# Gated linear attention in front of two MLPs: chunk decay moved onto q, weight splits moved to VectorE, y summed in two ways

## The chip, the cores and the metric

The kernel runs on one core of a Trainium2 chip. A core has TensorE (matrix products into PSUM; the profile calls its products PE and its weight loads PEld), VectorE (DVE), ScalarE (ACT), GpSimd (POOL) and SyncE (SP, here only a queue for transfers). The metric is device time in microseconds for one execution, and smaller is better.

## The reference

Shapes are batch 4, 8 heads, 768 positions and head width 48. The attention's output goes as 3072 tokens of 384 numbers through two MLPs in turn, with hidden widths 1536 and 2048. All inputs are 32-bit floats.

```python
f = 1.0 / (1.0 + np.exp(-f_logit))
for t in range(S):
    state = f[:, :, t, :, None] * state + np.einsum('bhd,bhe->bhde', k[:, :, t], v[:, :, t])
    y[:, :, t] = np.einsum('bhd,bhde->bhe', q[:, :, t], state)
# y as (3072 tokens, 384) is x of the first MLP, whose result is x of the second
gate = 1.0 / (1.0 + np.exp(-(x @ w_gate)));  x = gate * (x @ w_val) @ w_out
h = x @ w_in;  out = h * (1.0 / (1.0 + np.exp(-1.702 * h))) @ w_out
```

## The kernel before

**Attention in chunks.** The work is cut into 48 units. A unit is two heads and 256 positions, in four chunks of 64 positions. `Unit(n).third` says which third of the 768 positions it is, and a first third has no state ahead of it. For each unit the gates are multiplied up within a chunk (`prod`), q is multiplied by that product (`q_dec`) and k by its reciprocal (`k_dec`). Then y of a chunk is the masked scores `q_dec` times `k_dec` applied to v, plus `q_dec` times the state that stood ahead of the chunk. `p_end` is the product at a chunk's last position.

**Visits.** TensorE does the attention in 53 visits of small products. A visit turns one unit (transposes `k_dec` and makes its scores), makes the products of k and v of the unit before it (`kept`, at KV_COL of the banks), and makes y of the unit before that (`made`): the scores' part at Y_COL, the states' part at STATE_COL. Eight visits (BEFORE_MLP) stand ahead of the first MLP block; there both parts of y are summed in PSUM at Y_COL, which needs a wait of TensorE for its own earlier products (`tiles_done`). The other 45 stand inside MLP blocks, as the table VISIT_AT says: in blocks 1, 2, 4, 6, 8 of group 0 and in blocks 0, 1, 3, 4, 5, 7, 8, 9 of groups 1 to 5. PREPARE_AT does the same for the making of `prod`, its reciprocal, `q_dec` and `k_dec`, and FORGET_AT for the gates.

**MLP blocks.** The first MLP runs over seven groups of tokens: groups 0 and 1 have 256 tokens, the others 512, and each has 12 blocks of 128 hidden units. Each product is made as three, of parts that are rounded to fp32r (`w_hi`, `x_hi`) and of remainders (`w_lo`, `x_lo`), so every weight has to be split once. For block q, TensorE makes the gate (bank 0 of `up_ps`) and the value (bank 1), then the visit, if the block has one, and then the output product of block q-1. ScalarE takes the sigmoid of the gate (line 695), VectorE multiplies it by the value (line 891), ScalarE rounds that (`act_hi`, line 701) and VectorE takes the remainder (`act_lo`, line 900). Bank 0 of the next block waits for the sigmoid, bank 1 for the product, and the output product waits for the remainder. The second MLP follows in six groups of 512 tokens and 16 blocks each.

**Order.** Every engine runs an order that is written out by hand. In a block with a visit, VectorE goes on with `after_visit`: the mask of the scores (line 802), then `new_states`, which first multiplies all four chunks' k and v products by `p_end` from PSUM (line 812, it releases `kv_done`) and then adds the decayed state chunk by chunk (line 820). ScalarE in that block copies `k_rows` (line 616), takes y (`take_y`: four copies of the states' part, line 630, and one of the scores' part, line 633), makes the gates of a later unit (`forget`, lines 597 and 598) and, in group 0, rounds a piece of the first MLP's weights (line 578). GpSimd makes `q_dec` and `k_dec` (lines 509 and 514), adds the two parts of y (line 534) and splits the odd pieces 3, 5, 7, 9 and 11 of the weights (line 528); VectorE splits pieces 1, 2, 4, 6, 8 and 10 (line 842). SyncE's queue loads q, k, v and the gates' inputs and moves y into `x_raw` (line 402), from which the next group's x is split.

## Time and profile before

| | us |
|---|---|
| median of 3 runs | 967.32 |
| the runs | 965.22, 967.32, 1544.05 |
| the profiled execution, its own time | 964.99 |
| its span in the trace | 963.3 |
| TensorE busy | 934.1 (97%) |
| VectorE busy | 493.7 (51%) |
| ScalarE busy | 349.5 (36%) |
| GpSimd busy | 152.4 (16%) |

All times of rows are microseconds from the start of the span. In the rows of a timeline come start, duration, engine, line, operation, tile written and tiles read, and in brackets how long the engine had been idle and what ended it. Small matrix products overlap on TensorE, so its busy time is no measure of a full array. The columns of a window are its length, then the busy time and count of PE, PEld, DVE, ACT and POOL, then the granted share of TensorE's clock, the share of the DMA engines and their GB/s. The windows below are cut at the starts of VectorE's product of gate and value (line 891): 36.48, 44.24 and 90.27 are those of blocks 1, 2 and 10 of group 0; 95.82 and 142.66 those of blocks 0 and 10 of group 1; 181.94 and 189.57 those of blocks 4 and 5, and 197.19 and 203.31 those of blocks 6 and 7 of group 2. 149.43 is the first product of group 2.

### The profile page before, as it was taken

The numbers are of one execution on the slowest core, as the hardware profiler recorded it, in microseconds if no ns is written. First come the engines' busy times: TensorE is split into PE (matmuls) and PEld (weight loads), VectorE is DVE, ScalarE is ACT, GpSimd is POOL, SyncE is SP. The second block draws the span as 40 slices with busy tenths as digits, with TensorE's granted clock in tenths as the row PEclk, the third lists the DMA queues.
The fourth block names the chain that finished last, engine by engine and source line by source line (L and its number), as shares of the span: only waits on it lengthen the run. The fifth ranks groups of instructions, "written<-read, shape, count | busy, mean of one in ns | idle before, by whom it ended". The sixth has DMA issues, their size and how long they took to land.

```text
span 963.3 us, 18025 instructions
## 1 busy us (share of the span) xinstructions
PE 934.1 (97%) x7219; PEld 781.0 (81%) x7219; DVE 493.7 (51%) x872; ACT 349.5 (36%) x797; POOL 152.4 (16%) x174
## 2 busy tenths in 40 slices
PE   7888998999999999999999999999999999999997
PEld 5777897888888888888888888888888888888885
DVE  8976867655655765565333234343343443443433
ACT  3454453343434433333324333333332233233332
POOL 4443332221221221112004430000000000000000
PEclk9989999999999999999999999999999999999999
DMA  6642232211221211121032330020010100100000
GB/s 162 181 141 67 74 81 70 59 44 43 75 62 51 67 52 52 44 71 30 21 107 68 97 115 1 1 66 0 1 66 1 54 13 1 65 1 1 33 1 35
DMA packets 44007, 52.35 MB, mean 54 GB/s; under 512 B 8464, under 2 KB 33808, under 8 KB 43920
## 3 DMA queue, kind: packets, MB, share of 16 engines
q1 hardware_dynamic: 41184, 43.30, 15.5%
q10 hardware_dynamic: 2736, 7.85, 2.8%
q8 instruction: 59, 0.97, 0.4%
q14 instruction: 28, 0.23, 0.1%
HBM read 36.96 MB, written 9.44 MB: 48 GB/s over the span
## 4 chain that ended last, share of the span: by engine, by line
PE 85%; DVE 6%; issue 3%; ACT 2%; SPq 2%; DMA 1%; POOL 0%; ACTq 0%; DVEq 0%; POOLq 0%
PE up_ps L1052 16%; PE up_ps L1054 16%; PE up_ps L1053 16%; PE out_ps L1052 12%; PE out_ps L1053 11%; PE out_ps L1054 11%; PE att_ps L1003 1%; DVE prod L782 1%; SPq L402 1%; DVE act_lo L900 1%; DVE w_lo L842 1%; PE att_ps L1025 1%; PE att_ps L1045 1%; DVE inv_prod L789 1%; PE att_ps L1015 1%
## 5 line engine op out<-in xcount | busy, mean ns | idle before, releaser
L1052 PE MATMUL up_ps<-x_hi,w_hi 128*128 128x512 f32 (+1 forms) x792 | 295.1, 373 | 13.3 <-ACT act_f L695 12.1
L1054 PE MATMUL up_ps<-x_hi,w_lo 128*128 128x512 f32 (+1 forms) x792 | 294.5, 372 | 0.0
L1053 PE MATMUL up_ps<-x_lo,w_hi 128*128 128x512 f32 (+1 forms) x792 | 294.4, 372 | 0.0
L1052 PE MATMUL out_ps<-act_hi,w_hi 128*128 128x512 f32 (+1 forms) x540 | 208.6, 386 | 1.1 <-DVE act_lo L900 1.1
L1053 PE MATMUL out_ps<-act_lo,w_hi 128*128 128x512 f32 (+1 forms) x540 | 203.5, 377 | 0.0
L1054 PE MATMUL out_ps<-act_hi,w_lo 128*128 128x512 f32 (+1 forms) x540 | 203.1, 376 | 0.0
L701 ACT CAST act_hi<-act_f 128x512 fp32r<-128x512 f32 (+1 forms) x180 | 106.6, 592 | 249.6 <-DVE act_f L891 177.1
L900 DVE TENSOR_TENSOR act_lo<-act_f,act_hi 128x512 fp32r<-128x512 f32 (+1 forms) x180 | 126.1, 700 | 116.0 <-ACT act_hi L701 116.0
L1052 PEld LDWEIGHTS up_ps<-x_hi,w_hi 128*128 128x128 f32 x792 | 150.6, 190 | 40.1 <-issue 10.9
L1054 PEld LDWEIGHTS up_ps<-x_hi,w_lo 128*128 128x128 f32 x792 | 150.8, 190 | 25.4
L1053 PEld LDWEIGHTS up_ps<-x_lo,w_hi 128*128 128x128 f32 x792 | 150.8, 190 | 25.1
L894 DVE TENSOR_TENSOR act_f<-act_f,up_ps 128x512 f32<-128x512 f32 x96 | 66.1, 688 | 173.3 <-ACT act_f L697 173.3
L891 DVE TENSOR_TENSOR act_f<-act_f,up_ps 128x512 f32<-128x512 f32 (+1 forms) x84 | 51.2, 609 | 162.4 <-PE up_ps L1054 149.7
L697 ACT ACTIVATE act_f<-up_ps 128x512 f32<-128x512 f32 x96 | 57.4, 598 | 192.9 <-PE up_ps L1054 192.9
L1052 PEld LDWEIGHTS out_ps<-act_hi,w_hi 128*128 128x128 f32 x540 | 102.2, 189 | 22.8 <-DVE act_lo L900 1.8
L1054 PEld LDWEIGHTS out_ps<-act_hi,w_lo 128*128 128x128 f32 x540 | 102.3, 189 | 18.7
L1053 PEld LDWEIGHTS out_ps<-act_lo,w_hi 128*128 128x128 f32 x540 | 102.4, 190 | 17.0
L789 DVE RECIPROCAL inv_prod<-prod 128x256 f32<-128x256 f32 x48 | 84.1, 1753 | 1.6
L695 ACT ACTIVATE act_f<-up_ps 128x512 f32<-128x512 f32 (+1 forms) x84 | 45.0, 535 | 84.2 <-PE up_ps L1054 84.2
L630 ACT COPY y_t<-att_ps 48x128 f32<-48x128 f32 x176 | 45.8, 260 | 55.2 <-DVE state L812 53.6
L534 POOL TENSOR_TENSOR y_t<-y_t,y_scores 128x256 f32<-128x256 f32 x44 | 32.3, 734 | 210.4 <-ACT y_scores L633 210.4
L820 DVE SCALAR_TENSOR_TENSOR state<-state,p_end 128x48 f32<-128x48 f32 x176 | 47.7, 271 | 6.2
(77 smaller groups left out, 581.0 us busy)
## 6 DMA issues: line engine op xcount, KB each, us to landing
stage<-w SPq DMA_DIRECT2D x16, 384.0 KB, 3.3
stage<-w ACTq DMA_DIRECT2D x9, 576.0 KB, 4.3
q_raw<-q_t SPq DMA_DIRECT2D x96, 48.0 KB, 1.9
k_raw<-k_t SPq DMA_DIRECT2D x96, 48.0 KB, 1.9
v_raw<-v_n SPq DMA_DIRECT2D x48, 96.0 KB, 2.2
x_raw<-x_dram SPq DMA_DIRECT2D x6, 768.0 KB, 4.7
out_t<-final SPq DMA_DIRECT2D x18, 256.0 KB, 2.3
f_raw<-f_t SPq DMA_DIRECT2D x82, 48.0 KB, 1.9
```

The source lines that it names most:

```text
L630: act.copy(y[rows[i], :, r, :], banks(v)[rows[r], i, STATE_COL:STATE_COL + BLOCKS * C].rearrange("p (c t) -> p c t", c=BLOCKS))
L695: act.activation(act_f[:, b.t, 0:b.n], up_ps[:, 0, 0:b.n], ACT.Sigmoid).then_inc(sig_done, 1)
L697: act.activation(act_f[:, b.t, 0:b.n], up_ps[:, b.j % 2, 0:b.n], ACT.Sigmoid, scale=1.702).then_inc(sig_done, 1)
L701: act.copy(act_hi[:, b.t, 0:b.n], act_f[:, b.t, 0:b.n]).then_inc(act_hi_done, 1)
L789: dve.reciprocal(inv_prod[:, u.s, :], prod[:, u.s, :]).then_inc(inv_done, 1)
L820: dve.scalar_tensor_tensor(out=after[:, c, :], in0=state_before(u, c), scalar=p_end[:, n, c:c + 1], in1=after[:, c, :], op0=ALU.mult, op1= ...
L891: dve.tensor_tensor(act_f[:, b.t, 0:b.n], act_f[:, b.t, 0:b.n], up_ps[:, 1, 0:b.n], ALU.mult).then_inc(mul_done, 1)
L894: dve.tensor_tensor(act_f[:, b.t, 0:b.n], act_f[:, b.t, 0:b.n], up_ps[:, b.j % 2, 0:b.n], ALU.mult).then_inc(mul_done, 1)
L900: dve.tensor_tensor(act_lo[:, b.t, 0:b.n], act_f[:, b.t, 0:b.n], act_hi[:, b.t, 0:b.n].bitcast(F32), ALU.subtract).then_inc(act_split, 1)
L1052: pe.matmul(dst, w_hi[:, at:at + P], m_hi, start=first, stop=False)
L1053: pe.matmul(dst, w_hi[:, at:at + P], m_lo, start=False, stop=False)
L1054: return pe.matmul(dst, w_lo[:, at:at + P], m_hi, start=False, stop=last)
```

## The change

Four things change.

1. A state is now kept without the decay of its own chunk. `new_states` no longer multiplies the k and v products by `p_end`; each chunk's step reads them from PSUM and adds the state before it times the decay of the chunk before (`end_before`). The missing factor is put on q: ScalarE makes `q_in` from `q_dec`, chunk by chunk (`prepare_q`), and TensorE multiplies states by `q_in`. ScalarE also copies `p_end` now (`take_end`), which VectorE did.
2. VectorE splits all pieces of the first MLP's weights but the first; GpSimd's `split_w1_piece` goes.
3. For the visits of groups 0 and 1 (ahead of `APART`) TensorE sums both parts of y at Y_COL, as it did before the first block, behind its wait for `tiles_done`. ScalarE takes y in one copy, which no longer waits for VectorE; VectorE waits for that copy before it masks the scores (`copied_first`).
4. From group 2 on ScalarE makes the four copies of the states' part, once the states are done, and VectorE adds the scores' part from PSUM (`add_y`), where GpSimd did.

Some pieces of the order ahead of the first block are moved too: ScalarE rounds weight pieces 1 and 2 later, behind the copies of y and behind the first x; GpSimd makes unit 4's `k_dec` behind its last third of piece 0; SyncE loads the gates' input of unit 8 ahead of q and k of unit 7.

```diff
+
+    APART = VISIT_AT[2, 0]
...
+        def copied_first(v):
+
+            return BEFORE_MLP <= v < APART
 
         def wait_y(eng, n):
 
-            if out_visit[n] < BEFORE_MLP:
-                eng.wait_ge(y_taken, n + 1)
+            if out_visit[n] < APART:
+                eng.wait_ge(y_copied, n + 1)
             else:
-                eng.wait_ge(y_added, n - UG + 1)
+                eng.wait_ge(y_added, len([m for m in range(n + 1) if out_visit[m] >= APART]))
...
+        def end_before(u, c):
+
+            return p_end[:, u.n, c - 1:c] if c else p_end[:, u.n - UG, CH - 1:CH]
...
-                def split_w1_piece(t):
-
-                    piece = slice(t * PIECE1, (t + 1) * PIECE1)
-                    pool.wait_ge(w1_hi_done, t + 1)
-                    pool.tensor_tensor(w_lo[:, piece], w1_staged(t), w_hi[:, piece].bitcast(F32),
-                                       ALU.subtract).then_inc(w1_pool_split, 1)
-
-                def add_y(n):
-
-                    pool.wait_ge(y_taken, n + 1)
-                    pool.tensor_tensor(y_t[:, n % YS, :], y_t[:, n % YS, :], y_scores[:, n % 2, :], ALU.add).then_inc(y_added, 1)
...
-                pool.wait_ge(state_done, states_before(2))
+                pool.wait_ge(state_done, CH * 2)
                 split_w1(0)
                 split_w1(1)
-                decay(4)
+                decay_q(4)
+                pool.wait_ge(state_done, CH * 4)
                 split_w1(2)
+                decay_k(4)
...
                 for g in range(NG1 - 1):
                     for j in range(J1):
-                        if g == 0 and j + 2 < J1 and by_pool(j + 2):
-                            split_w1_piece(j + 2)
-                        if (g, j) in VISIT_AT and VISITS[VISIT_AT[g, j]][2] is not None:
-                            add_y(VISITS[VISIT_AT[g, j]][2])
                         if (g, j) in PREPARE_AT:
+                def take_end(n):
+
+                    act.wait_ge(scan_done, n + 1)
+                    act.copy(p_end[:, n, :],
+                             prod[:, n % 2, :].rearrange("p (c t) -> p c t", c=CH)[:, :, C - 1]).then_inc(p_end_done, 1)
+
+                def prepare_q(n):
+
+                    u = Unit(n)
+                    act.wait_ge(q_dec_done, n + 1)
+                    if n >= 2:
+                        act.wait_ge(visit_done, out_visit[n - 2] + 1)
+                    act.wait_ge(p_end_done, n + 1)
+                    for c in range(0 if u.third else 1, CH):
+                        at = slice(c * C, (c + 1) * C)
+                        last = act.mul(q_in[:, n % 2, at], q_dec[:, n % 4, at], end_before(u, c))
+                    last.then_inc(q_in_done, 1)
+
                 def take_y(n):
                     v = out_visit[n]
                     act.wait_ge(visit_done, v + 1)
-                    wait_products_read(act, v)
+                    if not copied_first(v):
+                        wait_products_read(act, v)
                     wait(act, y_moved[n % YS], 16 * moves(n % YS, n))
-                    scores_part = banks(v)[:, :, Y_COL:STATE_COL].rearrange("p r (c t) -> p c r t", c=BLOCKS)
                     y = y_t[:, n % YS, :].rearrange("p (c r t) -> p c r t", c=BLOCKS, r=SIDES)
-                    if v < BEFORE_MLP:
-                        act.copy(y, scores_part).then_inc(y_taken, 1)
+                    if v < APART:
+                        act.copy(y, banks(v)[:, :, Y_COL:STATE_COL].rearrange("p r (c t) -> p c r t", c=BLOCKS)).then_inc(y_copied, 1)
                         return
                     for i in range(PAIR):
                         for r in range(SIDES):
-                            act.copy(y[rows[i], :, r, :], banks(v)[rows[r], i, STATE_COL:STATE_COL + BLOCKS * C].rearrange(
+                            last = act.copy(y[rows[i], :, r, :], banks(v)[rows[r], i, STATE_COL:STATE_COL + BLOCKS * C].rearrange(
                                 "p (c t) -> p c t", c=BLOCKS))
-                    wait(act, y_added, n - 1 - UG)
-                    act.copy(y_scores[:, n % 2, :].rearrange("p (c r t) -> p c r t", c=BLOCKS, r=SIDES),
-                             scores_part).then_inc(y_taken, 1)
+                    last.then_inc(y_copied, 1)
...
+                    turned = made = None
                     if b.first_mlp and (b.g, b.j) in VISIT_AT:
                         turned, _, made = VISITS[VISIT_AT[b.g, b.j]]
-                        if turned is not None:
-                            take_k(turned)
-                        if made is not None:
-                            take_y(made)
+                    if turned is not None:
+                        take_k(turned)
+                        take_end(turned)
+                    if made is not None:
+                        take_y(made)
+                    if turned is not None:
+                        prepare_q(turned)
...
                     after = states_of(u)
-                    dve.tensor_tensor(after.rearrange("p (c r) e -> p r c e", r=SIDES),
-                                      banks(v)[:, :, KV_COL:Y_COL].rearrange("p r (c e) -> p r c e", c=BLOCKS),
-                                      p_end[:, n, :].rearrange("p (c r) -> p r c", r=SIDES).unsqueeze(3).to_broadcast(
-                                          [P, SIDES, BLOCKS, D]), ALU.mult).then_inc(kv_done, 1)
-                    dve.wait_ge(kv_done, n + 1)
-                    for m, c in enumerate(range(0 if u.third else 1, CH)):
-                        if m:
-                            dve.wait_ge(state_done, states_before(n) + m)
-                        dve.scalar_tensor_tensor(out=after[:, c, :], in0=state_before(u, c), scalar=p_end[:, n, c:c + 1],
-                                                 in1=after[:, c, :], op0=ALU.mult, op1=ALU.add).then_inc(state_done, 1)
+                    for c in range(CH):
+                        products = banks(v)[:, c % SIDES, KV_COL + c // SIDES * D:KV_COL + (c // SIDES + 1) * D]
+                        if c:
+                            dve.wait_ge(state_done, CH * n + c)
+                        if c == 0 and not u.third:
+                            dve.tensor_copy(after[:, c, :], products).then_inc(state_done, 1)
+                        else:
+                            dve.scalar_tensor_tensor(out=after[:, c, :], in0=state_before(u, c), scalar=end_before(u, c),
+                                                     in1=products, op0=ALU.mult, op1=ALU.add).then_inc(state_done, 1)
+
+                def add_y(n, v):
+
+
+                    dve.wait_ge(y_copied, n + 1)
+                    y = y_t[:, n % YS, :].rearrange("p (c r t) -> p r c t", c=BLOCKS, r=SIDES)
+                    dve.tensor_tensor(y, y, banks(v)[:, :, Y_COL:STATE_COL].rearrange("p r (c t) -> p r c t", c=BLOCKS),
+                                      ALU.add).then_inc(y_added, 1)
 
                 def after_visit(v):
                     turned, kept, made = VISITS[v]
                     dve.wait_ge(visit_done, v + 1)
+                    if made is not None and copied_first(v):
+                        wait_y(dve, made)
                     if turned is not None:
                         mask(turned, v)
                     if kept is not None:
                         new_states(kept, v)
+                    if made is not None and v >= APART:
+                        add_y(made, v)
...
                         if before[1] is not None:
-                            pe.wait_ge(kv_done, before[1] + 1)
+                            pe.wait_ge(state_done, CH * (before[1] + 1))
                         if before[2] is not None:
-                            pe.wait_ge(y_taken, before[2] + 1)
+                            wait_y(pe, before[2])
...
-                    if made is not None and v < BEFORE_MLP:
+                    if made is not None and v < APART:
 
                         last.then_inc(tiles_done, 1)
                         pe.wait_ge(tiles_done, made + 1)
-                        pe.wait_ge(state_done, states_before(made + 1))
+                        pe.wait_ge(state_done, CH * (made + 1))
+                        pe.wait_ge(q_in_done, made + 1)
                         for c in range(0 if m.third else 1, CH):
                             at = slice(Y_COL + c // SIDES * C, Y_COL + (c // SIDES + 1) * C)
                             for i in range(PAIR):
                                 last = pe.matmul(ps[rows[i], c % SIDES, at], state_before(m, c)[rows[i], :],
-                                                 q_dec[rows[i], made % 4, c * C:(c + 1) * C], start=False, stop=False,
+                                                 q_in[rows[i], made % 2, c * C:(c + 1) * C], start=False, stop=False,
                                                  skip_group_check=True)
                     elif made is not None:
 
-                        pe.wait_ge(state_done, states_before(made + 1))
+                        pe.wait_ge(state_done, CH * (made + 1))
+                        pe.wait_ge(q_in_done, made + 1)
                         for c in range(CH):
                             at = slice(STATE_COL + c // SIDES * C, STATE_COL + (c // SIDES + 1) * C)
+                            q = q_in[:, made % 2, c * C:(c + 1) * C] if m.third or c else q_dec[:, made % 4, 0:C]
                             for i in range(PAIR):
-                                last = pe.matmul(ps[rows[c % SIDES], i, at], state_before(m, c)[rows[i], :],
-                                                 q_dec[rows[i], made % 4, c * C:(c + 1) * C], start=False, stop=False,
+                                last = pe.matmul(ps[rows[c % SIDES], i, at], state_before(m, c)[rows[i], :], q[rows[i], :],
+                                                 start=False, stop=False,
```

The blocks 2 and 3 of group 0 on VectorE, from one product of gate and value to the last operation ahead of block 4's, in the kernel before:

```order
L891 TENSOR_TENSOR act_f<-act_f,up_ps 128x256
L842 TENSOR_TENSOR w_lo<-stage,w_hi 128x1152
L900 TENSOR_TENSOR act_lo<-act_f,act_hi 128x256
L802 TENSOR_TENSOR scores<-att_ps,causal 128x256
L812 TENSOR_TENSOR state<-att_ps,p_end 128x2x2x48
L820 SCALAR_TENSOR_TENSOR state<-state,p_end 128x48 x4
L891 TENSOR_TENSOR act_f<-act_f,up_ps 128x256
L900 TENSOR_TENSOR act_lo<-act_f,act_hi 128x256
L782 SCALAR_TENSOR_TENSOR prod<-gate,floor 128x256
L789 RECIPROCAL inv_prod<-prod 128x256
L790 COPY p_end<-prod 128x4
```

and in the changed kernel:

```order
L923 TENSOR_TENSOR act_f<-act_f,up_ps 128x256
L874 TENSOR_TENSOR w_lo<-stage,w_hi 128x1152
L932 TENSOR_TENSOR act_lo<-act_f,act_hi 128x256
L822 TENSOR_TENSOR scores<-att_ps,causal 128x256
L840 SCALAR_TENSOR_TENSOR state<-state,p_end,att_ps 128x48 x4
L923 TENSOR_TENSOR act_f<-act_f,up_ps 128x256
L874 TENSOR_TENSOR w_lo<-stage,w_hi 128x1152
L932 TENSOR_TENSOR act_lo<-act_f,act_hi 128x256
L804 SCALAR_TENSOR_TENSOR prod<-gate,floor 128x256
L811 RECIPROCAL inv_prod<-prod 128x256
```

The product of the states with `p_end` and the copy of `p_end` are gone, and block 3 has a split of a weight piece.

The same block 2 on ScalarE, from the rounding of `act_f` to the sigmoid of block 3, before:

```order
L701 CAST act_hi<-act_f 128x256
L616 COPY k_rows<-turn_ps 128x256
L630 COPY y_t<-att_ps 48x2x64 x4
L633 COPY y_scores<-att_ps 128x256
L597 ACTIVATE gate<-f_raw 128x4x63
L598 ACTIVATE floor<-f_raw 128x4
L578 CAST w_hi<-stage 128x1152
L572 DMA final<-w 128x1152
L695 ACTIVATE act_f<-up_ps 128x256
```

and changed:

```order
L718 CAST act_hi<-act_f 128x256
L607 COPY k_rows<-turn_ps 128x256
L612 COPY p_end<-prod 128x4
L635 COPY y_t<-att_ps 128x256
L624 ACTIVATE q_in<-q_dec,p_end 128x64 x4
L588 ACTIVATE gate<-f_raw 128x4x63
L589 ACTIVATE floor<-f_raw 128x4
L569 CAST w_hi<-stage 128x1152
L563 DMA final<-w 128x1152
L712 ACTIVATE act_f<-up_ps 128x256
```

Five copies of y have become one, and a copy of `p_end` and four products that make `q_in` stand behind it.

TensorE in the visit of block 2, with what each instruction waits for, before:

```order
L982 MATMUL turn_ps<-ident,k_dec 128x128 [waits k_rows_done,k_dec_done]
L982 MATMUL turn_ps<-ident,k_dec 128x128
L1003 MATMUL att_ps<-scores,v_raw 48x64 [waits scores_masked,kv_done]
L1003 MATMUL att_ps<-scores,v_raw 48x64 x7
L1015 MATMUL att_ps<-v_raw,k_rows 64x48 [waits v_loaded1,k_rows_done]
L1015 MATMUL att_ps<-v_raw,k_rows 64x48 x7
L1025 MATMUL att_ps<-q_dec,k_dec 64x64 [waits q_dec_done]
L1025 MATMUL att_ps<-q_dec,k_dec 64x64 x7
L1045 MATMUL att_ps<-q_dec,state 48x64 [waits state_done]
L1045 MATMUL att_ps<-q_dec,state 48x64 x7
```

and changed:

```order
L1014 MATMUL turn_ps<-ident,k_dec 128x128 [waits k_rows_done,k_dec_done]
L1014 MATMUL turn_ps<-ident,k_dec 128x128
L1035 MATMUL att_ps<-scores,v_raw 48x64 [waits scores_masked,state_done]
L1035 MATMUL att_ps<-scores,v_raw 48x64 x7
L1047 MATMUL att_ps<-v_raw,k_rows 64x48 [waits v_loaded1,k_rows_done]
L1047 MATMUL att_ps<-v_raw,k_rows 64x48 x7
L1057 MATMUL att_ps<-q_dec,k_dec 64x64 [waits q_dec_done]
L1057 MATMUL att_ps<-q_dec,k_dec 64x64 x7
L1069 MATMUL att_ps<-q_in,state 48x64 [waits q_in_done,state_done,tiles_done]
L1069 MATMUL att_ps<-q_in,state 48x64 x7
```

The last eight products now wait for TensorE's own earlier ones and for `q_in`, and the first ones for the finished states and not for `kv_done`.

## Rows read from the trace of the kernel before

**Rows 1.** The page, part 1: busy time, share of the span, instructions.

```profile
PE 934.1 (97%) x7219; PEld 781.0 (81%) x7219; DVE 493.7 (51%) x872; ACT 349.5 (36%) x797; POOL 152.4 (16%) x174
```

**Rows 2.** Windows: us; PE, PEld, DVE, ACT, POOL busy (count); PEclk; DMA; GB/s.

```profile
36.48:44.24 7.76, 5.18 (x87) 4.50 (x87) 7.11 (x12) 2.51 (x6) 4.08 (x4) 0.86 0.50 141
44.24:90.27 46.03, 36.87 (x418) 35.07 (x418) 34.74 (x58) 21.42 (x55) 19.46 (x16) 0.87 0.38 108
95.82:142.66 46.84, 45.04 (x801) 42.64 (x800) 35.87 (x85) 23.40 (x82) 14.45 (x20) 1.00 0.28 75
149.43:963.30 813.87, 807.78 (x5418) 665.85 (x5418) 375.73 (x649) 282.72 (x605) 96.06 (x106) 1.00 0.14 43
181.94:189.57 7.63, 7.63 (x95) 6.25 (x93) 5.43 (x12) 3.31 (x10) 2.17 (x3) 1.00 0.26 69
197.19:203.31 6.12, 6.12 (x29) 4.93 (x27) 3.76 (x5) 1.22 (x2) 1.47 (x2) 1.00 0.26 65
```

**Rows 3.** Timeline of VectorE, blocks 4 and 5: start, us, engine, line, operation.

```profile
55.75 0.42 DVE L891 TENSOR_TENSOR act_f<-act_f,up_ps 128x256 f32<-128x256 f32 x1
56.08 1.83 DVE L842 TENSOR_TENSOR w_lo<-stage,w_hi 128x1152 fp32r<-128x1152 f32 x1
57.83 0.41 DVE L900 TENSOR_TENSOR act_lo<-act_f,act_hi 128x256 fp32r<-128x256 f32 x1
58.17 0.41 DVE L802 TENSOR_TENSOR scores<-att_ps,causal 128x256 f32<-128x256 f32 x1
58.50 0.34 DVE L812 TENSOR_TENSOR state<-att_ps,p_end 128x192 f32<-128x192 f32 x1
58.87 1.18 DVE L820 SCALAR_TENSOR_TENSOR state<-state,p_end 128x48 f32<-128x48 f32 x4
...
63.12 1.80 DVE L900 TENSOR_TENSOR act_lo<-act_f,act_hi 128x256 fp32r<-128x256 f32 x1 [0.47 <-ACT act_hi L701]
64.85 0.68 DVE L782 TENSOR_TENSOR_SCAN prod<-gate,floor 128x256 f32<-128x256 f32 x1
65.56 1.75 DVE L789 RECIPROCAL inv_prod<-prod 128x256 f32<-128x256 f32 x1
```

**Rows 4.** Timeline of ScalarE in block 4, up to the sigmoid of block 5.

```profile
56.51 0.37 ACT L616 COPY k_rows<-turn_ps 128x256 f32<-128x256 f32 x1
59.00 1.08 ACT L630 COPY y_t<-att_ps 48x128 f32<-48x128 f32 x4 [2.12 <-DVE state L812]
...
60.68 0.20 ACT L598 ACTIVATE floor<-f_raw 128x4 f32<-128x4 f32 x1
60.77 1.14 ACT L578 CAST w_hi<-final 128x1152 fp32r<-128x1152 f32 x1
61.82 0.38 ACT L695 ACTIVATE act_f<-up_ps 128x256 f32<-128x256 f32 x1
```

**Rows 5.** Timeline of GpSimd in blocks 4 and 5.

```profile
55.95 0.74 POOL L514 TENSOR_TENSOR k_dec<-k_raw,inv_prod 128x256 f32<-128x256 f32 x1 [1.06 <-issue]
...
61.99 2.65 POOL L528 TENSOR_TENSOR w_lo<-final,w_hi 128x1152 fp32r<-128x1152 f32 x1 [0.72 <-ACT w_hi L578]
```

**Rows 6.** Timeline of weight loads at the third visit, ahead of the first block.

```profile
14.78 0.39 PEld L1036 LDWEIGHTS att_ps<-q_dec,state 48*48 48x48 f32 x12 [0.23 <-PE att_ps L1025]
```

**Rows 7.** Timeline of ScalarE while the first x comes in.

```profile
26.89 1.15 ACT L578 CAST w_hi<-stage 128x1152 fp32r<-128x1152 f32 x1 [2.25 <-DMA stage<-w]
```

**Rows 8.** Timeline of SyncE's queue at the end of group 1.

```profile
145.93 1.16 SPq L402 DMA_DIRECT2D x_raw<-y_t  x2
```

**Rows 9.** Timeline of ScalarE there: the last third of group 2's x.

```profile
148.47 0.62 ACT L647 CAST x_hi<-x_raw 128x512 fp32r<-128x512 f32 x1 [3.80 <-DMA x_raw<-y_t]
```

**Rows 10.** Timeline of TensorE there, groups 1 to 2.

```profile
146.47 0.28 PE L1053 MATMUL out_ps<-act_lo,w_hi 128*128 128x256 f32 x1
146.59 0.28 PE L1054 MATMUL out_ps<-act_hi,w_lo 128*128 128x256 f32 x1
149.43 0.50 PE L1052 MATMUL up_ps<-x_hi,w_hi 128*128 128x512 f32 x1 [2.56 <-ACT act_f L695]
```

52 lines of the change are left out of this document (29 added, 23 removed).

## The prediction

> **What bounds the kernel now.** I read the page's busy shares first, then windows cut at VectorE's product of gate and value, then the timelines of the engines inside one window. TensorE is busy 97% of the span [rows 1], so an edit elsewhere pays only where TensorE waits. The windows show where that is. From 149.43 us to the end TensorE is busy 807.8 of 813.9 us [rows 2]; there a block with a visit takes 7.63 us and one without 6.12, both fully busy, so a visit costs TensorE 1.51 us [rows 2]. A block of 256 tokens is 27 products that start 0.12 us apart [rows 10], 3.24 us. From 44.24 to 90.27 TensorE has eight such blocks and at most four visits, 8 x 3.24 + 4 x 1.51 = 32.0 us of work in a window of 46.03 us [rows 2]. That window, the one ahead of it (7.76 us) and the wait at 149.43 are where this change can move the end.
>
> Two blocks of group 0 take 46.03 / 4 = 11.5 us. The loop goes through VectorE and ScalarE. VectorE multiplies at 55.75, splits weights, takes the remainder at 57.83, masks, multiplies the k and v products by the decay, and starts the states at 58.87 [rows 3]. ScalarE can copy y only after that multiplication, at 59.00; then come 1.77 us of copies and gates and a weight cast of 1.05 us, so the next sigmoid starts at 61.82 [rows 4]. The product that follows it is 6.5 us behind the one at 55.75. In the next block VectorE's remainder takes 1.80 us, where the one before it left room for the mask after 0.34 [rows 3]: GpSimd was splitting a weight piece from 61.99 to 64.64 [rows 5], and the scan started at 64.85, when it was done.
>
> **Group 0, blocks 2 to 9.** I lay out the two blocks anew from the product M of the block with the visit. VectorE: weight split at M + 0.33, remainder at + 2.08, mask at + 2.42 [rows 3]. The multiplication of the k and v products is gone, so the four state steps start at + 2.75 and take 1.1 us, to + 3.85. They now read PSUM; the nearest row is the multiplication that did, 0.34 us for 192 elements, against 1.18 / 4 = 0.3 for a step of 48 [rows 3], so I add nothing, and 0.05 each at most. ScalarE: `k_rows` at + 0.76 [rows 4], then the copy of `p_end` (0.1), one copy of y (0.27), at + 1.4 the four products for `q_in`. No row shows these. From below they cost 0.1 each, the step from the small gate at 60.68 to the cast at 60.77; from above I take 0.5, twice a copy of y, which is 1.08 / 4 = 0.27 [rows 4]. I take 0.27, as small operations in a row with separate operands are nearest to it. Then gates 0.42 (1.77 less four copies and the fifth of 0.27), cast 1.05, sigmoid 0.4 [rows 4]: the next product comes at + 4.4, and ScalarE, not VectorE's + 3.85, paces it.
>
> The Trainium skill, "ScalarE: Activation LUTs", section "What ACT_TABLE_LOAD costs", says that each operand given as a pointer of one element a partition adds about 93 ns to an ACTIVATE, and that ACTIVATEs in a row overlap by as much; that makes an estimate of 0.24 us for each of the four, and 0.1 us less per two blocks than my sum. No row here shows it.
>
> The second block has no visit: product 0.33, split 1.2, remainder 0.34, scan 0.70, reciprocal 1.7 [rows 3] = 4.25 us. The split is priced from the row at 56.08: it lasts 1.83 us, but GpSimd's `k_dec` ran until 55.95 + 0.74 = 56.69 [rows 5], and 57.91 - 56.69 = 1.2 is left. GpSimd does nothing at that point of the second block now, so 1.2 stands, and 1.83 is the bound from above. Sum 8.6 us against 11.5, and for four such pairs a gain of **11.6 us**. TensorE's floor, 2 x 3.24 + 1.51 + 0.23 (below) = 8.2, lies just under it, so no more than 13 can be had here.
>
> The Trainium skill, "SBUF — State Buffer", section "Who interferes with whom", speaks against moving such work: a VectorE instruction with two inputs in SBUF and a GpSimd instruction that reads SBUF lock each other out for a whole instruction. By that rule the new splits still collide with `q_dec` and `k_dec`, and if each of the five met one the four pairs would gain 9 and not 11.6. The trace agrees that there is such a collision (1.83 against 1.2, and 1.80 against a remainder's 0.41 [rows 3]), but those products follow the scan and the reciprocal, which in the second block come after the split.
>
> **Group 0, the ends.** Between the products of blocks 1 and 2 lie 7.76 us [rows 2], with the same stall by GpSimd. Laid out anew: 2.42 to the mask, 0.33, 1.1 of states, 0.7 of scan, 1.7 of reciprocal = 6.25, a gain of **1.5**. From block 10's product to the first one of group 1 there are 5.55 us [rows 2]; TensorE needs 0.42 until the product is done, four times 1.08 us, and 0.3 for the last to land, 5.05. The clock was below full for part of the window just before (mean 0.87), and with TensorE kept busy I expect it back: **0.5**.
>
> **Ahead of the first block.** ScalarE waited 2.25 us for a weight piece and only then copied `k_rows` and rounded x [rows 7]. The piece now comes behind x. But y is copied later, since for it the states must be finished, and the products for `q_in` lengthen ScalarE's way to the first sigmoid. I take **0.4** of gain, between a loss of 1 and a gain of 1.5 (the 1.15 us of the cast and a little of the wait).
>
> **Group 1.** Ten blocks and eight visits take 46.84 us [rows 2]. TensorE now waits for its own products in each visit. At a visit that already did, its weight load sat idle 0.23 us for that [rows 6]. Its floor becomes 10 x 3.24 + 8 x (1.51 + 0.23) = 46.3. VectorE's loop there loses the multiplication, which put 0.37 us ahead of the states [rows 3], and gains a wait for the copy of y ahead of the mask: with no split in the block the mask could start 1.2 us behind the product, and ScalarE, by the layout above, is through with y at about 1.55, 0.35 later. So blocks with a visit and a preparation stay as long as they are, and those with a visit alone get shorter, since ScalarE comes to the next sigmoid earlier. The floor binds: **0.5**, with 0 to -5 if the two waits add up (rival 2). At its end TensorE is through its products at 146.7 and starts group 2 at 149.43, 2.56 us idle [rows 10]: ScalarE's third rounding of x waited until 148.47 for a transfer [rows 9] that SyncE issued at 145.93, without a pause behind the one before it [rows 8], so the queue itself was late. Each y is ready about 2.6 us earlier now: 1.1 for four copies of the five, 0.7 for GpSimd's sum (priced as `k_dec` [rows 5]), 0.8 for ScalarE's wait for VectorE. A queue that fills up behind y ends about as much earlier. VectorE's split of x then follows its reciprocal, which keeps 0.7 us: **1.9**.
>
> **Groups 2 to 5** have 32 visits. GpSimd's sum goes, VectorE's comes. VectorE's blocks: scores at 2.42 less 0.34 behind the remainder plus 0.65 for 512 columns, states done at about 3.4 from the product, wait 1.1 for ScalarE's four copies, sum 0.34, scan 0.7, reciprocal 1.7: 7.3 us in a block of 7.63. It fits, TensorE stays full, and nothing moves. If that cover is gone, see rival 3. The rest has no edit.
>
> **Sum.** 0.4 + 1.5 + 11.6 + 0.5 + 0.5 + 1.9 = 16.4 us from the profiled execution's 964.99 (span 963.3): 948.6. The two ordinary runs lie 0.2 and 2.3 above that execution, so for a median I take **949.5**. About 2%, 19.3 us, is what a measurement of this kernel can tell from no change.
>
> **Rivals.** (1) ScalarE and GpSimd pace group 0. If the four products take 0.5 each, the next product comes at + 5.3 and the pair at 9.5 us: the gain shrinks by 3.6, and with every split locked out by GpSimd, 1.83 in both blocks, by 2.5 more, to about 10.3: 955.5. For it: its chain holds 3.9 us of the 4.4 already. Against: a gate of 4 columns costs it 0.1. (2) In group 1 VectorE's wait for the copy (0.35) and TensorE's own wait (0.23) come in series, eight times, 4.6 us, and 0.5 is not gained: 11.3 in all, 954.5. For it: both engines are within 0.5 us of each other there. (3) The other side: groups 2 to 5. VectorE's 7.3 us rest on a wait for ScalarE. If copies, `q_in` and sum cost 0.8 us more a visit than counted, a block takes 8.1, 0.5 over TensorE's, and 32 visits give back 16: 965.5. At 1.4 more it is 984, slower than before. It decides from 7.63 us on, and only if the blocks without a visit don't catch up; TensorE runs 4.9 us (1.51 + 2 x 2.04 - 0.7) behind the product before it feels it, which speaks against it. (4) Both loops reach TensorE's floor and the start gains its 1.5: 13 + 1.5 + 1.5 + 0.5 + 0.5 + 2.6 = 19.6: 945.5. (5) The change doesn't do what it says in group 0: the sigmoid stays late because the early copy of y waits for a visit that TensorE ends late, and only the stalls by GpSimd go (1.8 - 0.4 less the split's 1.2): next to nothing there, 963.
>
> **How the numbers follow.** Forecast 0.58 (946.5 to 952.5), rival 1 0.12, rival 2 0.09, rival 3 0.04 (0.03 over 2%), rival 4 0.15, rival 5 0.02. The range 945 to 957.5 takes in the forecast, 1, 2 and 4 with the bounds of the unknown costs, and leaves out 3, 5 and tails of the others. Faster by over 2% needs 948.0 or less against the median, which rival 4 gives and the forecast's lower end against one reading of the two runs: 0.25. Slower by over 2%: 0.03. Within: 0.72.
>
> **What would show it.** The pair of blocks in group 0 at 8.6 us (8.2 if TensorE binds, 9.5 if rival 1); no remainder of 1.8 us on VectorE; `q_in` products near 0.3 us; group 1's window at 46 to 47 and not 50; the idle ahead of group 2 below 0.8; blocks of group 2 still 7.63 and 6.12; the clock at 2.4 GHz through most of group 0. The forecast is wrong if TensorE waits in groups 2 to 5, or if the first product of group 0 starts more than 1 us from 31.3.

## The result: 953.13 us, 13 us less than before

The changed kernel takes 953.13 us (median of five, 952.64 to 954.03), the kernel before 966.21 beside it; the ratio of the two is 0.9868, with a 95% interval of 0.9852 to 0.9883. That is a gain of 1.3%, inside the 2% that was set for "no change", and 3.6 us above the forecast of 949.5. One of the five executions of the kernel before stood at 1544 us; the median counts it, the ratio leaves it out. The profiled execution took 953.08 us with a span of 951.0, against 964.99 and 963.3.

The page of the changed kernel, part 1 [beside rows 1]:

```profile
PE 934.9 (98%) x7203; PEld 781.2 (82%) x7203; DVE 487.0 (51%) x829; ACT 375.3 (39%) x941; POOL 105.8 (11%) x125
```

VectorE has 7 us less to do, ScalarE 26 more, GpSimd 47 less, and TensorE the same. So the 12.3 us between the spans are waits of TensorE that are gone. Where they were is seen in windows of the changed kernel, cut at VectorE's product of gate and value as in [rows 2] (columns: us; busy us and count of PE, PEld, DVE, ACT, POOL; granted clock; DMA share; GB/s):

```profile
0.00:34.60 34.60, 27.18 (x354) 20.66 (x354) 25.02 (x45) 17.03 (x53) 13.13 (x25) 0.95 0.64 178
...
39.05:45.27 6.22, 4.66 (x89) 4.24 (x88) 6.08 (x12) 3.57 (x11) 1.47 (x2) 0.96 0.57 161
45.27:79.52 34.25, 33.99 (x425) 32.84 (x424) 32.36 (x53) 21.27 (x59) 5.85 (x8) 0.96 0.51 146
...
84.84:132.68 47.84, 47.14 (x785) 44.21 (x784) 33.62 (x75) 22.89 (x86) 8.80 (x12) 1.00 0.31 82
132.68:137.08 4.40, 4.21 (x36) 4.03 (x35) 3.89 (x6) 2.25 (x5) 1.29 (x2) 1.00 0.25 66
137.08:951.00 813.92, 808.04 (x5418) 665.86 (x5418) 379.08 (x630) 303.74 (x715) 73.22 (x75) 1.00 0.15 43
```

Set against the windows of before, this is the whole account:

```
stretch                                   before   after   gain   forecast
start to the first product                 31.72   34.60   -2.9      0.4
product of block 0 to 1                     4.76    4.45    0.3      0
product of block 1 to 2                     7.76    6.22    1.5      1.5
blocks 2 to 10 of group 0 (four pairs)     46.03   34.25   11.8     11.6
block 10 to group 1                         5.55    5.32    0.2      0.5
group 1, ten blocks, eight visits          46.84   47.84   -1.0      0.5
to TensorE's start of group 2               6.77    4.40    2.4      1.9
groups 2 to 5, and the rest               813.87  813.92    0        0
sum                                                        12.3     16.4
```

A pair of blocks now takes 34.25 / 4 = 8.56 us. That is a mean: in the first block of the four pairs TensorE's clock was granted at 0.67 and the block took 4.45 us,

```profile
45.27:49.72 4.45, 4.45 (x29) 4.45 (x28) 3.80 (x9) 3.73 (x12) 0.73 (x1) 0.67 0.40 103
```

and the other three pairs took 8.49 us (4.16 behind the block with the visit, 4.33 behind the other). In the run with one slab in the gap, below, the clock was full in all four pairs, and they took 33.96 us, 8.49 each. VectorE's timeline in blocks 6 and 7 [beside rows 3]:

```profile
62.54 0.36 DVE L923 TENSOR_TENSOR act_f<-act_f,up_ps 128x256 f32<-128x256 f32 x1
62.82 1.88 DVE L874 TENSOR_TENSOR w_lo<-stage,w_hi 128x1152 fp32r<-128x1152 f32 x1
64.62 0.41 DVE L932 TENSOR_TENSOR act_lo<-act_f,act_hi 128x256 fp32r<-128x256 f32 x1
64.95 0.41 DVE L822 TENSOR_TENSOR scores<-att_ps,causal 128x256 f32<-128x256 f32 x1
65.29 1.15 DVE L840 SCALAR_TENSOR_TENSOR state<-state,p_end,att_ps 128x48 f32<-128x48 f32 x4
66.70 0.42 DVE L923 TENSOR_TENSOR act_f<-act_f,up_ps 128x256 f32<-128x256 f32 x1 [0.26 <-ACT act_f L712]
67.04 1.35 DVE L874 TENSOR_TENSOR w_lo<-stage,w_hi 128x1152 fp32r<-128x1152 f32 x1
...
```

The multiplication of the k and v products is gone, and so is the remainder of 1.80 us. VectorE idles 0.26 us in the pair, where ScalarE's sigmoid comes last. The second split meets no GpSimd instruction and takes 1.35 us; the first meets `k_dec` and takes 1.88. ScalarE's timeline in the same pair [beside rows 4]:

```profile
63.24 0.37 ACT L607 COPY k_rows<-turn_ps 128x256 f32<-128x256 f32 x1
...
63.61 0.38 ACT L635 COPY y_t<-att_ps 128x256 f32<-128x256 f32 x1
63.87 0.36 ACT L624 ACTIVATE q_in<-q_dec,p_end 128x64 f32<-128x64 f32 x1
...
64.12 0.82 ACT L624 ACTIVATE q_in<-q_dec,p_end 128x64 f32<-128x64 f32 x3
64.84 0.41 ACT L588 ACTIVATE gate<-f_raw 128x252 f32<-128x252 f32 x1
...
65.24 1.15 ACT L569 CAST w_hi<-stage 128x1152 fp32r<-128x1152 f32 x1
66.28 0.39 ACT L712 ACTIVATE act_f<-up_ps 128x256 f32<-128x256 f32 x1
```

y is copied 1.07 us behind the product, where it was 3.25 [rows 3, 4], in one copy and not five. TensorE's list of waits says the same. Of the kernel before (engine, line, what is waited for: us in total, times, longest):

```profile
PE up_ps L1052 <- ACT act_f L695: 12.1, 7, 2.7
```

and of the changed one:

```profile
PE out_ps L1035 <- DVE state L840: 2.4, 1, 2.4
...
PE up_ps L1087 <- ACT act_f L712: 0.6, 1, 0.6
```

The 12.1 us take in the 2.56 us ahead of group 2 [rows 10]. The wait of 2.4 us stands ahead of the first block. It is longer than before and not new: in the same visits of the kernel before TensorE waited 0.80 us for the copy of y (at 20.89) and 0.23 and 0.41 us for states (at 21.57 and 22.75), 1.4 us in all. ScalarE's timeline there, where y of pairs 0 to 3 is copied at 18.32, 22.34, 24.67 and 25.96 (17.14, 20.27, 22.15 and 24.28 in the kernel before):

```profile
18.32 0.37 ACT L635 COPY y_t<-att_ps 128x256 f32<-128x256 f32 x1 [0.98 <-DVE state L840]
...
18.95 0.83 ACT L624 ACTIVATE q_in<-q_dec,p_end 128x64 f32<-128x64 f32 x3
19.68 0.40 ACT L588 ACTIVATE gate<-f_raw 128x252 f32<-128x252 f32 x1
...
22.34 0.37 ACT L635 COPY y_t<-out_ps 128x256 f32<-128x256 f32 x1 [2.16 <-DVE state L838]
```

VectorE's scan of that gate stands ahead of its mask of the fourth visit (its second row is the mask of 20.82):

```profile
20.21 0.69 DVE L804 TENSOR_TENSOR_SCAN prod<-gate,floor 128x256 f32<-128x256 f32 x1 [2.00 <-ACT floor L589]
20.82 0.40 DVE L822 TENSOR_TENSOR scores<-out_ps,causal 128x256 f32<-128x256 f32 x1
```

SyncE moves y into x, one transfer behind the other, from the second copy of y on: from 22.74 and not from 20.85. And TensorE ran at half its clock for a while: the 16 small products that fill the time ahead of pair 4's transposition took 2.05 us in the kernel before (granted clock 1.00),

```profile
23.22 2.05 PE L967 MATMUL up_ps<-ident 128*128 128x128 f32 x16
```

and in the changed kernel, with 0.50 from 25.0 to 27.0 (1.2 GHz),

```profile
25.16 3.25 PE L999 MATMUL up_ps<-ident 128*128 128x128 f32 x16
```

### The profile page after: what moved, and what is told of

The parts are those of the page before. It is cut to its first block, busy times and chain, and to the rows that moved or that the text cites. A ratio compares the mean times of both kernels' runs of the same rounds, so it can differ in the third digit from the quotient of the medians.

```text
span 951.0 us, 18139 instructions
## 1 busy us (share of the span) xinstructions
PE 934.9 (98%) x7203; PEld 781.2 (82%) x7203; DVE 487.0 (51%) x829; ACT 375.3 (39%) x941; POOL 105.8 (11%) x125
## 4 chain that ended last, share of the span: by engine, by line
PE 95%; DVE 2%; issue 1%; ACT 1%; DMA 1%; SPq 0%; ACTq 0%; POOL 0%; DVEq 0%; POOLq 0%
PE up_ps L1087 17%; PE up_ps L1088 17%; PE up_ps L1089 17%; PE out_ps L1087 13%; PE out_ps L1088 12%; PE out_ps L1089 12%; PE att_ps L1035 2%; PE att_ps L1057 1%; PE att_ps L1047 1%; PE turn_ps L1014 1%; PE up_ps L1003 1%; PE att_ps L1069 1%; PE att_ps L1080 1%; DMA x_raw<-y_t 1%; DVE inv_prod L811 1%
## 5 line engine op out<-in xcount | busy, mean ns | idle before, releaser
L932 DVE TENSOR_TENSOR act_lo<-act_f,act_hi 128x512 fp32r<-128x512 f32 (+1 forms) x180 | 118.1, 656 | 113.8 <-ACT act_hi L718 113.8
L506 POOL TENSOR_TENSOR q_dec<-q_raw,prod 128x256 f32<-128x256 f32 x48 | 35.3, 735 | 299.6 <-DVE prod L804 229.9
L639 ACT COPY y_t<-att_ps 48x128 f32<-48x128 f32 x128 | 33.3, 260 | 60.3 <-DVE state L840 59.2
L624 ACT ACTIVATE q_in<-q_dec,p_end 128x64 f32<-128x64 f32 x176 | 47.4, 339 | 0.9
```

The source lines that it names most:

```text
L506: pool.tensor_tensor(q_dec[:, n % 4, :], q_raw[:, u.s, :], prod[:, u.s, :], ALU.mult).then_inc(q_dec_done, 1)
L624: last = act.mul(q_in[:, n % 2, at], q_dec[:, n % 4, at], end_before(u, c))
L932: dve.tensor_tensor(act_lo[:, b.t, 0:b.n], act_f[:, b.t, 0:b.n], act_hi[:, b.t, 0:b.n].bitcast(F32), ALU.subtract).then_inc(act_split, 1)
```

## The experiments

The theory after the result had four parts. (1) The early copy of y carries the gain of group 0, since it takes VectorE's work out of ScalarE's way. (2) The splits' move carries a small part of it. (3) The 2.9 us lost at the start come of the order of ScalarE's queue. (4) Group 1 loses 1.0 us to TensorE's wait for its own products. The rivals stand with each run. The runs bear out (1), and (2) with a size of 0.7 us a pair. They bear out (3) only in part and (4) only in part, as is said where they stand.

**Splits back on GpSimd.** The diff against the changed kernel; `split_w1_piece`, `by_pool` and the semaphore are as in the kernel before:

```
+                        if g == 0 and j + 2 < J1 and by_pool(j + 2):
+                            split_w1_piece(j + 2)
...
-                    if b.q < J1 and b.j + 2 < J1:
+                    if b.q < J1 and b.j + 2 < J1 and not by_pool(b.j + 2):
```

> The changed kernel with one part undone: every second split of a weight piece goes back to GpSimd. Theory A (a GpSimd split stops VectorE's two-input instructions while it runs, so moving it to VectorE is part of the gain): GpSimd's 2.65 us from about 0.3 us ahead of the product hold up the remainder and the scan of the second block of each pair; the pair goes from 8.56 to about 9.3, and blocks 1 to 2 from 6.22 to 7: 957 against 953.1. Theory B (the split's owner doesn't matter, only the multiplication of the k and v products and the four copies did): VectorE has 1.35 us less in a pair whose two blocks take 4.16 and 4.33, TensorE's 8.3 binds: 952, 1 us less. In both the start and group 1 stay as they are, within 0.5.

Measured: 954.08 us (953.34 to 954.4). Four pairs took 36.78 us, 9.20 each. The timelines of GpSimd, and then of VectorE, in the second block of a pair:

```profile
66.52 2.68 POOL L540 TENSOR_TENSOR w_lo<-stage,w_hi 128x1152 fp32r<-128x1152 f32 x1 [2.97 <-ACT w_hi L585]
```

```profile
67.65 1.84 DVE L948 TENSOR_TENSOR act_lo<-act_f,act_hi 128x256 fp32r<-128x256 f32 x1 [0.47 <-ACT act_hi L734]
```

The remainder of 1.84 us is back; GpSimd's split ends at 69.20 and the remainder at 69.49. Theory A in mechanism and in the length of the pair. The pairs are 2.5 us longer than in the changed kernel's profile, and 2.8 us, 0.7 a pair, longer than four pairs of 8.49. The time rose by 1.0 us and not by 4: the pairs cost 2.5 and not 3, blocks 1 to 2 nothing (6.03 us) where I expected 0.8, and this execution's first product came 0.8 us earlier, for a reason that the table below shows.

**Gates first.** ScalarE's order ahead of the first block:

```
+                forget(4)
                 w1_first_part(0)
                 take_y(0)
                 take_end(3)
                 take_k(3)
-                load_w1(1)
                 prepare_q(2)
-                forget(4)
-                take_y(1)
-                prepare_q(3)
+                load_w1(1)
                 first_load_f(6)
                 load_w1(2)
                 forget(5)
+                prepare_q(3)
+                take_y(1)
                 take_y(2)
```

> The changed kernel with ScalarE's order ahead of the first block changed: the gate of pair 4 ahead of the rounding of the first weight piece and of the copy of y of pair 0, and the gate of pair 5, the load of f of pair 6, the load of weight piece 2 and q_in of pair 3 ahead of the copy of y of pair 1. Theory A (the first block starts 2.9 us later than before because ScalarE's q_in products and the later copies of y stand ahead of a gate whose scan in turn stands ahead of VectorE's mask): the mask of the fourth visit comes at about 20.0 instead of 20.8, TensorE's wait of 2.38 us at 22.97 falls below 1.7, the copies of y of pairs 2 and 3 at about 23.3 and 24.5 instead of 24.67 and 25.96, and the first product at 33.1 to 33.4 instead of 34.60: 951.4 to 952. Theory B (it is late because y needs the finished states and the warm-up ended 1.2 us later in that execution; the gates only fill time): the first product stays at 34.3 to 34.7 and the time at 953.

Measured: 952.01 us (950.4 to 952.3), first product at 33.72. The mask came at 19.33, but y of pair 1 was copied at 21.83, behind the gate and `q_in` that I had moved ahead of it, and TensorE waited 2.29 us for that copy. Part of theory A: the early gate gave the mask its time back, and the new order gave it away one row on. And 33.72 lies among the first products that executions of the changed kernel's own order gave (32.67 to 34.60, table below), so a gain from this order isn't shown.

**One slab in the gap.** In group 1 TensorE issues three products of the block before between a visit's products and its wait for them:

```
                         last.then_inc(tiles_done, 1)
+                        if between is not None:
+                            between()
                         pe.wait_ge(tiles_done, made + 1)
...
-                        out(BLOCK[q - 1])
+                        out(BLOCK[q - 1], range(1 if early else 0, KC))
```

> The changed kernel, with TensorE's wait for its own products in the eight visits of group 1 covered: the three products of the first slab of the block before are issued between the last of the visit's products and the wait. Nothing is left out. Theory A (the wait stands alone, 0.36 us a visit, since TensorE paces group 1): a block with a visit goes from 5.11 to about 4.8, the window of ten blocks from 47.84 to 45.5 and 45: 950.5. Theory B (the 0.36 us is what it costs to change from tiles to whole-array products, or VectorE paces these blocks anyway): the window stays at 47.5 to 48.5 and the time at 953 or a little more.

Measured: 952.38 us (952.04 to 953.4); the window of group 1 took 48.16 us, a block with a visit 5.15. Theory B. TensorE's timeline in a visit of the changed kernel (the products before these, of `att_ps` from `v_raw` and `k_rows`, start at 117.64):

```profile
117.86 0.43 PE L1057 MATMUL att_ps<-q_dec,k_dec 48*64 48x64 f32 x16
118.38 0.54 PE L1069 MATMUL att_ps<-q_in,state 48*48 48x64 f32 x12
118.85 0.39 PE L1087 MATMUL out_ps<-act_hi,w_hi 128*128 128x256 f32 x1
119.07 0.28 PE L1088 MATMUL out_ps<-act_lo,w_hi 128*128 128x256 f32 x1
```

and the same with the slab in the gap:

```profile
116.66 0.43 PE L1057 MATMUL att_ps<-q_dec,k_dec 48*64 48x64 f32 x16
117.02 0.39 PE L1089 MATMUL out_ps<-act_hi,w_hi 128*128 128x256 f32 x1
117.24 0.28 PE L1090 MATMUL out_ps<-act_lo,w_hi 128*128 128x256 f32 x1
117.36 0.29 PE L1091 MATMUL out_ps<-act_hi,w_lo 128*128 128x256 f32 x1
117.57 0.54 PE L1071 MATMUL att_ps<-q_in,state 48*48 48x64 f32 x12
118.04 0.39 PE L1089 MATMUL out_ps<-act_hi,w_hi 128*128 128x256 f32 x1
```

Sixteen small products follow each other in 0.22 us (117.64 to 117.86). With the wait the next group comes 0.52 behind, 0.3 more. In the second trace the wait is covered, but the large products come 0.36 behind the small ones (0.14 more), the second large one 0.22 behind the first (0.1 more than 0.12), and the small ones 0.21 behind the last large one (0.09 more). So in this visit the change between the two shapes of product cost in both directions together (0.33) what the wait did (0.30), and hiding the wait behind products of the other shape gained nothing. VectorE is not what held the block there, for these rows of TensorE follow each other without a wait for it.

What the sum on TensorE costs is more than this wait. In a visit of group 1 in the kernel before, where the states' part has columns of its own:

```profile
96.34 0.43 PE L1025 MATMUL att_ps<-q_dec,k_dec 48*64 48x64 f32 x16
96.59 0.40 PE L1045 MATMUL att_ps<-q_dec,state 48*48 48x64 f32 x16
96.92 0.38 PE L1052 MATMUL out_ps<-act_hi,w_hi 128*128 128x256 f32 x1
```

There the group starts 0.25 us behind the one before it, 0.27 sooner than the 0.52 with the wait, and its 16 products take 0.33 us to the next large one. With both parts summed at Y_COL 12 products take 0.47 us to it (118.38 to 118.85), and 16 take 0.58 (85.88 to 86.46, in the first four visits of the group). A block with a visit took TensorE 4.7 us there and takes 5.11 or 5.23 here: 0.27 of that is the wait, the rest is in these products. Why they are slower no run shows.

**Group 1's y by VectorE.** `APART = VISIT_AT[1, 0]` in place of `VISIT_AT[2, 0]`.

> The changed kernel with group 1's y summed by VectorE as in groups 2 to 5 (states' part in columns of its own, four copies by ScalarE, a sum by VectorE), so TensorE's own wait is gone there. Theory A (with 256 columns a block VectorE paces if it also waits for four copies): blocks with a visit and a preparation take 6.6 us, ten blocks 52 to 53 instead of 47.84: 957.5 to 958.5. Theory B (TensorE paces group 1, VectorE catches up in the blocks without a visit, and TensorE's wait for itself is what the sum on TensorE costs): 10 x 3.24 + 8 x 1.51 = 44.5, so 950.

Measured: 961.72 us (961.16 to 962.92); the window of group 1 took 58.49 us instead of 47.84. Theory A's mechanism, and twice its price. VectorE's timeline in a block with a visit and a preparation:

```profile
111.88 0.42 DVE L848 TENSOR_TENSOR y_t<-y_t,att_ps 128x256 f32<-128x256 f32 x1 [1.27 <-ACT y_t L639]
```

and ScalarE's:

```profile
110.77 1.07 ACT L639 COPY y_t<-att_ps 48x128 f32<-48x128 f32 x4 [1.60 <-DVE state L840]
111.87 0.82 ACT L624 ACTIVATE q_in<-q_dec,p_end 128x64 f32<-128x64 f32 x3
...
113.13 0.38 ACT L712 ACTIVATE act_f<-up_ps 128x256 f32<-128x256 f32 x1
```

108.00 to 114.61 is the 6.6 us expected. What I had too low is the block with a visit alone, 4.8: the products stand 5.5 to 5.8 us apart there, since ScalarE reaches the sigmoid by way of the states, four copies and `q_in`; and among the blocks with a preparation one took 7.1 and the first of the group 7.7 (7.0 in the changed kernel). Summing on TensorE, some 0.4 to 0.5 us a visit, is the cheap way.

**Both small groups' y by VectorE.** `APART = BEFORE_MLP`.

> The changed kernel with y of both small groups summed by VectorE, as in groups 2 to 5 (beside group 1 of the run before this one, group 0 too). Theory A (in group 0 ScalarE's copies then come behind VectorE's states and stand ahead of q_in, gate, cast and sigmoid): product + 3.85 for the states, 1.08 for four copies, 1.06 for q_in, 0.42, 1.05 and 0.4 make 7.9 instead of 4.16 to the next product, and VectorE's sum 0.34 in the second block: a pair of about 12.5 instead of 8.56, 961.7 + 16 = 975 to 979, slower than before. Theory B (GpSimd's split and the multiplication were the cost, where y is summed matters little in group 0): a pair of at most 9.5, 962 to 966.

Measured: 978.19 us (977.26 to 978.95), a ratio of 1.0132 to the kernel before (1.0115 to 1.0149). Four pairs took 49.77 us, 12.44 each: theory A to 0.1. The scheme of groups 2 to 5, put into the small groups, makes the kernel slower than before.

**y copied late.** `copied_first` returns False, so that ScalarE copies y only when the states are done; the summing on TensorE stays.

> The changed kernel in which ScalarE copies y in groups 0 and 1 only when VectorE has read the visit's products (scores masked, states done), as the rule for all other visits is; nothing else changes. Theory A (the early copy of y carries the gain of blocks 2 to 9, because it takes VectorE's work out of ScalarE's way to the next sigmoid): the copy comes at product + 3.9 instead of + 1.07, the next product at + 7.0 instead of + 4.16, a pair takes 11.3 instead of 8.56, and group 1 gains or loses under 2: 964 to 967. Theory B (the gain is VectorE's: no multiplication, no stall by GpSimd's split; ScalarE has room): a pair stays below 9.2: 953 to 956.

Measured: 963.4 us (961.91 to 964.72). Four pairs took 45.95 us, 11.49 each, group 1 48.09. ScalarE's timeline in one of these pairs:

```profile
70.27 0.37 ACT L635 COPY y_t<-att_ps 128x256 f32<-128x256 f32 x1 [2.91 <-DVE state L840]
...
71.91 1.14 ACT L569 CAST w_hi<-stage 128x1152 fp32r<-128x1152 f32 x1
72.95 0.38 ACT L712 ACTIVATE act_f<-up_ps 128x256 f32<-128x256 f32 x1
```

The product stood at 66.20, the next at 73.36, 7.16 behind. A pair is as long as in the kernel before (11.51), with all other parts of the change in place. Theory A. The pairs alone give 11.7 us of the 11.8. The time is 0.6 us below the range expected; in its profiled execution the first product came at 32.67. But this run does not put the kernel before's wait back. There the copy waited for the multiplication by `p_end` and came 3.25 us behind the product; here it waits for the finished states and comes 4.07 behind. So the 3.0 us (11.49 less 8.49) are the price of a copy behind the states, and 2.2 of them (3.25 less 1.07) are the gain of the early copy over the kernel before.

**The splits alone,** in the kernel before: all of them by VectorE.

> The kernel before with one part of the change alone: all splits of weight pieces by VectorE. Theory A (ScalarE's late copy of y paces the first block of a pair, 6.5 us, whatever GpSimd does; only the second block changes, from 5.02 to 0.33 + 1.35 + 0.34 + 0.7 + 1.7 = 4.4 us, and blocks 1 to 2 from 7.76 to about 7.0): 4 x 0.6 + 0.7 = 3 us, 962 to 963 against 965.4. Theory B (the stall by GpSimd is what the change mainly removes): a pair of 9.5 or less, 957. Theory C (a split by VectorE costs the block what the stall did): 965.

Measured: 961.81 us (961.22 to 963.23), ratio 0.9958 (0.9941 to 0.9975). Four pairs took 43.36 us, 10.84 each, blocks 1 to 2 6.62. Theory A: the first block of a pair stayed at 6.5 (65.74 to 72.22), the second shrank from 5.0 to 4.35. So this part gives 0.67 us a pair by itself, and 0.7 where the rest is in place (first run). With that the pair's gain is laid open. In the block with the visit the copy comes 2.18 us sooner (3.25 to 1.07), and from the copy to the next product go 3.09 us where 3.23 went (6.48 less 3.25), since the copies that are gone make up for `q_in`: 0.14. The other block is 0.7 shorter. The sum is 3.02, and the pair went from 11.51 to 8.49.

**y of pair 1 first.** The order with the gates first, changed once more:

```
                 load_w1(2)
+                take_y(1)
                 forget(5)
                 prepare_q(3)
-                take_y(1)
```

> The order of the run with the gates first, but with the copy of y of pair 1 ahead of the gate of pair 5 and of q_in of pair 3. In the run with the gates first VectorE had finished the states at 20.77 and ScalarE copied y only at 21.83, behind these four and behind three issues of transfers; TensorE waited 2.29 us for that copy at 22.43, and SyncE's six moves of y into x, one behind the other from 22.20, are what the first x waits for. Theory A: the copy comes at 20.8, TensorE goes on at 21.3, the first move at 21.2, and the first product comes 1.0 us earlier than with the gates first, 2.0 us earlier than in the changed kernel for the same landing of the first f (q_dec of pair 2 at 10.8: 32.3 to 32.6): 950.8 to 951.5. Theory B (weight piece 2 and its rounding, or the transfer of x itself, come last): 33.3 to 33.7, and 952.

Measured: 950.97 us (950.18 to 951.41). The row that decides, of ScalarE, and the first move of SyncE:

```profile
20.53 0.37 ACT L635 COPY y_t<-out_ps 128x256 f32<-128x256 f32 x1 [1.55 <-DVE state L838]
```

```profile
21.23 3.71 SPq L401 DMA_DIRECT2D x_raw<-y_t  x6
```

TensorE's wait for states fell from 2.4 to 1.4 us, as theory A says, and the copies of y of pairs 1 to 3 came 1.0, 1.6 and 1.7 us earlier than in the first run with a like start (20.53, 22.26, 23.56 against 21.54, 23.86, 25.01). The first product came at 32.96, 0.9 us earlier and not 2.0. ScalarE waited 1.68 us for the transfer of x, rounded the last of it by 30.24, and came to the sigmoid at 32.57: theory B for the rest. The copies are shown to come earlier. That the kernel is faster for it is not: 32.96 lies among the first products of the changed kernel's order, and the ratio to the kernel before, 0.9846 (0.9829 to 0.9862), overlaps with the changed kernel's.

**Short queues, and a later weight piece,** beside the changed kernel once more. The first moves `prepare_q(4)` behind block 0's rounding and changes VectorE's order:

```
                 begin_decay(5)
+                end_decay(5)
                 w1_second_part(1)
-                x_second_part(0)
                 after_visit(7)
-                end_decay(5)
+                x_second_part(0)
```

The second also puts `load_w1(3)` behind `take_k(4)`.

> The changed kernel itself once more, beside the two below on one chip. Both theories: 953 to 953.5; the first product between 33.8 and 34.6, by when the scan of pair 2 gets its gate (q_dec of pair 2 at 10.8 to 11.6).

> The kernel with y of pair 1 first, and two more moves ahead of the first product: ScalarE makes q_in of pair 4 after the first block's rounding and not ahead of its sigmoid, and VectorE takes the reciprocal of pair 5 right behind its scan and the mask of pair 4 ahead of the split of x. Theory A (behind the x both queues are what is late: there ScalarE rounded x until 30.2 and came to the sigmoid at 32.57 by way of a cast of 1.15, q_in 1.06 and a gate 0.5, VectorE was in the reciprocal until 32.6): sigmoid at 31.5, first product at 32.0 to 32.2 instead of 32.96, 950.0 to 950.3. Theory B (the product only moves the wait to the next split or to the visit of block 1, where pair 4 is late): first product earlier, but the product of block 2 stays at 43.6 and the time at 951.

> The same, and ScalarE issues the load of weight piece 3 (0.59 MB) behind k_rows of pair 4, at about 27.1 instead of 24.55, so that it does not share the DMA engines with the last moves of y into x. Theory A (those moves took from 24.4 to 29.5 in the kernel with y of pair 1 first, and 3.1 us in the kernel before, because of this load): x lands 1 us earlier, the first product at 31.2 to 31.5, 949.3. Theory B (the moves share with SyncE's loads of k, q, v and with piece 2, or the piece itself comes too late for its rounding at 34.1): no gain over the run without it, or a loss of up to 1.

Measured: the changed kernel 952.29 us (950.87 to 953.15, ratio 0.9857, 0.9841 to 0.9872), the short queues 951.21 (949.28 to 953.32, ratio 0.9858, 0.9838 to 0.9877), with the later piece 950.76 (949.61 to 951.35, ratio to before 0.9843, 0.9829 to 0.9857). The profiled executions ahead of the first product (us; "x rounded" is the end of ScalarE's third rounding):

```
kernel               first      y of pair 1  16 filler  k_rows     x         sigmoid  first
                     transpos.  copied       products   of pair 4  rounded            product
before                 8.23       20.27        2.05      27.95      29.23     30.57    31.72
splits alone           9.43       20.91        3.60      28.80      30.08     31.89    33.04
changed                9.52       22.34        3.25      28.66      31.88     34.21    34.60
changed, again         9.44       22.25        3.20      28.53      31.81     34.14    34.53
splits on GpSimd       8.64       21.54        3.78      29.14      30.42     32.75    33.84
slab in the gap        8.44       21.53        3.78      29.23      30.52     32.84    33.83
group 1 by VectorE     8.71       21.55        3.78      29.39      30.67     33.00    34.06
both by VectorE        8.38       21.53        3.78      29.17      30.46     32.78    33.76
y copied late          9.02       21.83        2.86      28.08      29.70     32.03    32.67
gates first            9.07       21.83        2.97      28.05      31.00     33.33    33.72
y of pair 1 first      8.49       20.53        3.07      26.77      30.24     32.57    32.96
short queues           8.35       20.52        2.83      26.76      28.76     30.21    31.36
short, later piece     8.16       20.55        3.78      28.16      29.66     31.71    32.87
```

The kernels from "changed" to "y copied late" are one program up to the first product, and so are the first two. Still their first products lie between 32.67 and 34.60, and between 31.72 and 33.04. Two things differ between executions: when TensorE is through its first warm-up products (first column), and how long the clock is at half speed while the 16 filler products run (third). Those stand ahead of pair 4's transposition, whose copy `k_rows` stands ahead of the rounding of x on ScalarE. The means are 32.4 and 33.9, so of the 2.9 us that the two profiled executions show, about 1.5 belong to the change. The means are of two and of seven executions, and the ranges touch, so the size is rough. The times give another measure of it: the other stretches gave 15.2 us and the medians 13.1 and 13.5, which leaves a loss of 1.7 to 2.1.

Two parts of it can be seen. y of pair 1 is copied 1.3 us later (21.53 against 20.27, at like starts). And ScalarE takes 2.33 us from the last rounding of x to the sigmoid in every one of the changed programs down to "y of pair 1 first": the cast of weight piece 2 (1.15 us), four products for `q_in` (1.06) and a gate. In the kernel before and with the splits alone these were 1.34 and 1.81 us, of which it waited 0.92 and 1.39 for TensorE. But this second part set the first product only where x came late: in both profiles of the changed kernel, with the gates first and with y of pair 1 first. In the other five executions of the changed order (down to "y copied late") VectorE had the sigmoid and waited 0.5 to 0.9 us for TensorE's value product, so there TensorE, with its late and slow fillers, came last.

With short queues ScalarE's way was 1.45 us, and the first product came at 31.36: theory A in its profile, though 0.6 to 0.8 us more than expected, since x was there at 28.4. Its theory B fell there too, for the product of block 2 came at 41.91 and not at 43.6. But that profile is of the fastest of four executions (949.28, 950.07, 952.35 and 953.32), and the median, 951.21, is theory B's 951 and not theory A's 950.0 to 950.3. So the shorter way is shown, and a gain in time is not. With the later weight piece the fillers took 3.78 us at half clock and `k_rows` came at 28.16; ScalarE then found x there without a wait, so that run can't tell what the load does to the transfer. In time the three orders lie within 0.5 us of each other, and single executions of one of them 4.0 us apart. Their medians are 1 to 2 us below the changed kernel's, but the intervals of their ratios all overlap with its own, and the ratio of the short queues is the same. That one of them is faster isn't shown, and which is best stays open.

**q_in by GpSimd.** `prepare_q` as one or two GpSimd products with `p_end` spread over the columns, ahead of the next decay:

```
+                    if u.third:
+                        pool.tensor_tensor(q[:, 0, :], q_d[:, 0, :], end_before(u, 0).to_broadcast([P, C]), ALU.mult)
+                    pool.tensor_tensor(q[:, 1:CH, :], q_d[:, 1:CH, :],
+                                       p_end[:, n, 0:CH - 1].unsqueeze(2).to_broadcast([P, CH - 1, C]),
+                                       ALU.mult).then_inc(q_in_done, 1)
```

> The changed kernel with q_in made by GpSimd in one or two products of 192 and 64 columns, in place of three or four by ScalarE (nothing left out). Theory A (ScalarE paces the first block of a pair and the start, so its 1.06 us of q_in count): the product behind a visit comes 3.9 us (VectorE's own work: 1.88, 0.34, 0.34, 1.15, 0.4) instead of 4.16 behind the one before, the pair goes from 8.56 to TensorE's 8.3, and the first block starts 0.8 to 1.5 us earlier: 950.5 to 951.5. Theory B (GpSimd's products read SBUF while VectorE splits a weight piece, and each holds the other up): the split in the block with the visit grows from 1.88 to 2.4 or more, the pair to 9.0 or more, and the time is 953 to 956.

Measured: 952.28 us (950.9 to 953.76). In the three last pairs products stood 8.47 us apart, the one behind a visit 4.13 behind the one before (8.49 and 4.16 in the changed kernel). The first pair took 10.18, for its first block took 5.85 us at a granted clock of 0.55, fully busy on TensorE; four pairs took 35.58. The timelines of GpSimd and of VectorE in the last but one:

```profile
63.46 0.73 POOL L514 TENSOR_TENSOR k_dec<-k_raw,inv_prod 128x256 f32<-128x256 f32 x1 [1.05 <-issue]
64.58 0.97 POOL L531 TENSOR_TENSOR q_in<-q_dec,p_end 128x64 f32<-128x64 f32 x1 [0.39 <-ACT p_end L634]
```

```profile
63.52 1.88 DVE L877 TENSOR_TENSOR w_lo<-stage,w_hi 128x1152 fp32r<-128x1152 f32 x1
```

The product of 64 columns ran into VectorE's split, which stood from 63.52 to 65.40, and ended at 65.55; in group 1 such products took 0.29 us. The split is no longer than without it (1.88), and the remainder behind it took 0.51 instead of 0.41. So there is a collision, but GpSimd bore it and not VectorE, and theory B fell. Theory A is right in kind and tiny in size: with ScalarE relieved of 1.06 us, the pair gave 0.02. The first product came at 33.95, among those of the changed kernel: the fillers took 3.78 us, `k_rows` of pair 4 came at 29.26, and with `q_in` gone from its queue ScalarE only waited 0.79 us for TensorE at the sigmoid. So in such an execution `q_in` ahead of the sigmoid cost next to nothing.

## Why the prediction came out as it did

The range (945 to 957.5) held the time, and the forecast was 3.6 us low, just outside its own 946.5 to 952.5. Where the time fell is in part luck: the range reached so far up to make room for rivals 1 and 2, and neither of them came. The mechanism held in group 0, which gives 11.8 of the 12.3 us. One of the signs that the prediction named for being wrong did come: the first product started at 34.60, 3.3 us from 31.3, where 1 us was allowed.

**Blocks 2 to 9 of group 0**, 11.6 forecast, 11.8 measured. The pair was laid out at 8.6 and took 8.56, or 8.49 at full clock; ScalarE paces its first block and VectorE its second, as said. Two small misses cancel in it: the first block was laid out at 4.4 and took 4.16, the second at 4.25 and took 4.33, since a split that meets no GpSimd instruction takes 1.35 and not 1.2. The prediction had read the 1.2 as a difference of two rows, and no row showed it. The late copy and the splits alone show that both halves of the argument hold, and their sizes. `q_in` was priced 0.27 apiece. The rows give 0.24 (four in 1.06 us); a single one shows 0.34. The Trainium skill, "ScalarE: Activation LUTs", section "What ACT_TABLE_LOAD costs", led to the estimate of 0.24, and the trace agrees.

**The bound by GpSimd's collisions** (9 us in place of 11.6, by the Trainium skill's "SBUF — State Buffer", section "Who interferes with whom") didn't bind: the split in the block with the visit met `k_dec` (1.88 us), the other took 1.35, and GpSimd's `q_dec` in the second block ran beside the reciprocal. That the collision itself is real, the first run shows: 1.84 for a remainder that takes 0.42.

**Blocks 1 to 2, and the end of group 0**: 1.5 and 1.5; 0.5 and 0.2. The reason given for the 0.5, a clock that comes back, was wrong: the granted clock was 1.00 in that window before (90.27 to 95.82) and after.

**Group 1**: 0.5 of gain forecast, 1.0 of loss measured. The step that failed is the floor, which took a visit to be 1.51 us as before and added only TensorE's wait of 0.23 (the idle of a weight load [rows 6]). A block with a visit takes 5.11 us, so the sum on TensorE costs 5.11 - 3.24 - 1.51 = 0.36 (0.4 against the 4.7 us of such a block in group 1 before), and the floor is 47.4, not 46.3; the first four visits, with 16 products for the states' part and not 12, took 0.12 more. The wait itself was nearly right (0.27 to 0.30); left out was that the products behind it take longer to the next large one (0.47 or 0.58 us, where 0.33 went before). Rival 2, the two waits in series, did not come: its VectorE part stayed hidden. The slab in the gap shows that the wait is no idle time that products of the other shape could fill.

**The end of group 1**: 1.9 forecast, 2.4 measured; the first moves of the last y left SyncE at 131.92 and x was rounded without a wait at 133.45.

**Groups 2 to 5**: nothing moved, as said; VectorE's wait for ScalarE's four copies measured 1.27 and not 1.1, and TensorE didn't feel it.

**Ahead of the first block** is the largest miss, and a step that failed. It took a gain of 0.4, with a loss of 1 at worst; the two executions show a loss of 2.9, of which about 1.5 to 2 is the change's. It counted the cast of weight piece 2 as a gain of 1.15 us, "the piece now comes behind x", since ScalarE waited for it [rows 7]. But the changed kernel's ScalarE waits for x there (0.76 and 0.82 us in the profile), and behind x the cast stands ahead of the first sigmoid. It named the later copies of y and didn't follow them: the copy of pair 1 sets when SyncE's six moves begin, which are issued one behind the other for 3.7 to 4.6 us. Of the 4.1 us between forecast and measured spans 3.3 lie here, 1.5 in group 1, and the other stretches gave 0.7 more than forecast. The medians stand 13.1 and 13.5 us apart in the two comparisons, 0.8 to 1.2 more than the profiled spans.

## What to carry to other kernels

Where two in-order engines hand a tile to and fro, ask of each copy out of PSUM which of its waits it needs: one copy that no longer waited for the other engine gave 2.2 of the 3.0 us a pair, and with that copy behind the finished states all the rest of the change gave nothing in these blocks. Price a change of order ahead of a loop by following every queue to the loop's first instruction, transfers issued in a row included; and before a loss of 1 or 2 us at the start is put down to the change, look at the same stretch in several executions of the same program. A wait of TensorE between two groups of small products isn't free room for large ones.

## What the runs showed of the hardware

TensorE needs 0.3 us more where small products wait for the small ones before them, and about as much (0.14 + 0.1 + 0.09) for going to large products and back. The 16 small products behind such a wait, which add to columns that others have just written, took 0.58 us to the next large one, where 16 into columns of their own took 0.33. ScalarE's copies and products in a row start 0.1 us sooner than their length says: 0.34 alone, 0.24 in a row. A GpSimd product of 64 columns took 0.97 us where it started during VectorE's split, and 0.29 us in group 1, so a product of a third of the size can be the longer one (192 columns took 0.69 right behind it); VectorE's split was no longer for it. The start of one and the same program differed by 1.9 us between executions (32.67 to 34.60). In part that is the clock: in every profiled execution but one TensorE was granted 1.2 GHz for some time after its wait for pair 1's y or states, between about 22 and 29 us, and 16 filler products took 2.8 to 3.8 us in place of 2.05. The one exception is the kernel before. The run with the splits alone is the same program up to there and had the same waits (0.80, 0.23 and 0.41 us), and its fillers took 3.60 us; so the waits alone don't tell which it will be.
